# Clustered attention and two feed-forward layers on one core: moving the fourth product with V of each unit to the next step of TensorE

## What is computed

```python
# q, k, v: (2, 8, 768, 64); centroids: (8, 16, 64)
q_assign = argmax(einsum('bhsd,hcd->bhsc', q_n, c_n))      # nearest cluster of each query
k_assign = argmax(einsum('bhsd,hcd->bhsc', k_n, c_n))      # and of each key
mask = q_assign[:, :, :, None] == k_assign[:, :, None, :]
scores = where(mask, q @ k.T / sqrt(64), -1e9)
scores = scores - max(scores, axis=-1)
attn = exp(scores); attn = attn / (sum(attn, axis=-1) + 1e-9)
x = attn @ v                                               # then the two layers:
h = x @ w_in; g = P(h) / Q(h); y = g @ w_out               # moe,  d_ff = 2048
out = ((y @ w1) * (y @ w2)) @ w3 @ w_out                   # moe2, d_ff = 1024
```

## Time and profile before

| | us |
|---|---|
| median of 3 runs | 744.41 (744.14 to 745.87) |
| profiled execution, its time on the device | 743.99 |
| its span, first to last instruction | 742.2 |
| TensorE matmul busy | 721.5 (97%) |
| VectorE busy | 498.6 (67%) |
| ScalarE busy | 422.3 (57%) |
| GpSimd busy | 343.7 (46%) |
| TensorE's mean granted clock, share of full speed | 0.995 |

### The profile page before, as it was taken

The page is one execution under the profiler, slowest core; times in us unless marked ns, Lnnn a source line. Parts: engine busy times, 40 slices in busy tenths (PEclk is TensorE's granted clock), DMA queues, the critical chain, the costliest instruction groups (busy, mean ns, idle before and its releaser), DMA issues.

```text
span 742.2 us, 12733 instructions
## 1 busy us (share of the span) xinstructions
PE 721.5 (97%) x4849; PEld 591.2 (80%) x4849; DVE 498.6 (67%) x814; ACT 422.3 (57%) x750; POOL 343.7 (46%) x258
## 2 busy tenths in 40 slices
PE   4799999999999999999999999999999999999998
PEld 2467777777767788888888888878789999998886
DVE  6888888888855577677776777775876465543211
ACT  4366767666646888877767677764343322323221
POOL 5068787787875647642222224440204666451000
PEclk9899999999999999999999999999999999999999
DMA  7335645545421352000000032003101101000111
GB/s 159 72 89 129 157 112 150 145 114 151 104 55 39 115 162 68 0 1 1 0 1 1 0 114 103 11 29 89 54 30 29 30 29 56 2 1 23 49 43 57
DMA packets 66876, 47.75 MB, mean 64 GB/s; under 512 B 30528, under 2 KB 59136, under 8 KB 66816
## 3 DMA queue, kind: packets, MB, share of 16 engines
q1 hardware_dynamic: 66816, 46.95, 22.9%
HBM read 28.35 MB, written 3.15 MB: 42 GB/s over the span
## 4 chain that ended last, share of the span: by engine, by line
PE 91%; DVE 3%; SPq 2%; ACT 2%; DMA 1%; issue 1%; POOL 0%; DVEq 0%; ACTq 0%
PE psum L1156 89%; PE psum L1161 1%; DVE psum L1673 1%; DVE MROW L1673 1%; PE psum L688 1%; SPq L1095 1%; DVE OPS L1608 1%; DMA BQS<-NMT 1%; DMA RAWQK<-in_k 0%; ACT P L1452 0%; SPq L1078 0%; SPq L1055 0%; ACT OPS L1416 0%; DVE YS L884 0%; PE psum L1234 0%
## 5 line engine op out<-in xcount | busy, mean ns | idle before, releaser
L556 POOL TENSOR_TENSOR G<-TT,G 128x512 fp32r<-128x512 f32 x47 | 61.1, 1301 | 150.0 <-ACT G L435 150.0
L1838 POOL TENSOR_TENSOR PSUMS<-PSUMS,P 128x768 f32<-128x768 f32 x64 | 108.3, 1692 | 17.0 <-ACT P L1452 9.0
L1452 ACT ACTIVATE P<-psum 128x768 f32<-128x768 f32 x96 | 76.3, 809 | 46.5 <-PE psum L1156 46.1
L1673 DVE TENSOR_REDUCE psum<-psum 128x1 f32<-128x768 f32 x90 | 86.4, 960 | 19.7 <-PE psum L1156 18.8
L1156 PE MATMUL psum<-G,WSPLIT 128*128 128x512 f32 x360 | 86.8, 390 | 0.3 <-POOL G L556 0.3
L1156 PE MATMUL psum<-XT,WSPLIT 128*128 128x512 f32 x360 | 86.5, 389 | 0.0
L483 DVE SCALAR_TENSOR_TENSOR HH<-UU,ABSB,psum 128x512 f32<-128x512 f32 x48 | 35.9, 748 | 69.0 <-ACT TT L413 69.0
L1156 PEld LDWEIGHTS psum<-G,WSPLIT 128*128 128x128 f32 x360 | 67.3, 188 | 15.2 <-POOL G L556 0.9
L1156 PEld LDWEIGHTS psum<-XT,WSPLIT 128*128 128x128 f32 x360 | 67.6, 188 | 14.0
L1156 PE MATMUL psum<-P,V 128*32 128x194 f32 x1536 | 76.0, 332 | 0.1
L1156 PE MATMUL psum<-XT,SW 128*128 128x384 f32 x384 | 71.7, 334 | 0.0
(11 more groups left out here) (134 smaller groups left out, 1408.1 us busy)
## 6 DMA issues: line engine op xcount, KB each, us to landing
W3R<-in_moe_w SPq DMA_DIRECT2D x8, 512.0 KB, 3.7
RAWF<-in_moe_w SPq DMA_DIRECT2D x16, 256.0 KB, 3.3
RAWQK<-in_q SPq DMA_DIRECT2D x16, 192.0 KB, 3.2
RAWQK<-in_k SPq DMA_DIRECT2D x16, 192.0 KB, 3.9
BQS<-OPS SPq DMA_DIRECT2D x16, 192.0 KB, 2.8
OPS<-OPS SPq DMA_DIRECT2D x16, 192.0 KB, 3.0
V<-in_v SPq DMA_DIRECT2D x16, 192.0 KB, 2.6
XT<-XH SPq DMA_DIRECT2D x64, 48.0 KB, 2.0
```

Of the source, the lines that this page charges most:

```text
L556: nc.gpsimd.tensor_tensor(G[:, n % 2, 1, :], TT[:, n % 4, :], G[:, n % 2, 0, :].bitcast(F32), ALU.subtract).then_inc(g_lo, 1)
L1452: nc.scalar.activation(P32[:, (2 * u + n) % 4, :, 0:QS].rearrange("p (x y) n -> p x y n", x=2), score_banks(u, n).rearrange("p x (y n) -> ...
L1673: nc.vector.tensor_reduce(rows[:, n:n + 1], maxima_banks(u, n), AX.XY, ALU.max).then_inc(sm_free, 1)
L1838: nc.gpsimd.tensor_tensor(total, P32[:, (2 * u) % 4, :, 0:QS] if n == 1 else total, P32[:, (2 * u + n) % 4, :, 0:QS], ALU.add).then_inc(p_ ...
```

## The change

In TensorE's list, `probs_v(u, 3)` leaves the end of step u. It is issued in step u+1 instead, behind `scores(u + 1, 0)` and `score_max(u + 2, 3)` and directly in front of `probs_v(u, 4)`. For the last step its place is behind `scores(14, 0)`. No other engine's list is edited, and no wait, operand or size.

```diff
@@ -1338,6 +1338,8 @@
             def step(u):
                 scores(u, 0)
                 score_max(u + 1, 3)
+                if u > 1:
+                    probs_v(u - 1, 3)
                 probs_v(u - 1, 4)
                 probs_v(u - 1, 5)
                 sums(u - 1)
@@ -1359,12 +1361,12 @@
                 if has(u + 4):
                     sides(u + 4)
                 score_max(u + 2, 2)
-                probs_v(u, 3)
 
             for u in range(1, UNITS - 2):
                 step(u)
 
             scores(14, 0)
+            probs_v(13, 3)
             probs_v(13, 4)
             probs_v(13, 5)
             score_max(15, 3)
```

## The result

| | before | after |
|---|---|---|
| median of 6 runs, us | 744.47 (743.83 to 745.87) | 748.92 (747.94 to 751.73) |
| profiled execution, us | 743.99 | 749.49 |
| its span, us | 742.2 | 747.7 |

The ratio is 1.0059, with a 95% interval of 1.0049 to 1.0070: the change makes the kernel 4.45 us slower. Lines of the code behind the edit have moved by one or two: the reduction of `row_max` is L1675 now, the transpose of `turn_one_hot` L1670.

What follows compares the result with a forecast made beforehand. TensorE, busy 97% of the span, was taken to bound the kernel. Eleven boundaries at 0.30, plus 0.67, less 0.30 gave +3.67 us; 747.66 from the profiled run, forecast as 748.1 us, range 745.2 to 750.0.

Steps and rivals of the forecast that it cites:

- The new stretch: TensorE from score_max(u+2, 2) to sums(u): forecast 4.21 us against 3.91, so 0.30 us slower in each step.
- The chain by step 1: Step 1 already has this adjacency: 1.68 us between its two score_max, against 1.66 forecast for the new order.
- Part 1: TensorE's stretch to sums(u): grouping like products saves switches of shape, 3.61 us for 3.91, gaining 0.30 us a step.
- Part 2: At score_max(u+2, 3): the reduction loses its cover, so TensorE waits 0.50 us and restarts 0.10 us slower.
- The late landing: At scores(u+1, 0): one boundary in twelve has a late maxima DMA, taken to recur and cost 0.67 us.
- The last boundary: Step 13 to scores(14, 0): switches saved with no reduction in the way, -0.30 us.
- the eleven others: The boundaries without a late maxima DMA, each forecast to lose 0.30 us.
- The first: Rival at row_max(u+2, 2): the reduction doesn't bind, only switches count; 3.9 us won, 740.5 us; chance 0.08.
- the second: Rival at the same wait: it exists but is smaller; +1.0 to +2.2 us, 745.4 to 746.6; chance 0.17.
- The third: Rival at scores(u+1, 0): the maxima's DMA becomes the bound at every boundary; +7.7 us, 752.1; chance 0.06.
- the fourth: Rival on TensorE's clock: stalls lower it to 8 tenths, about 42 us, near 790; chance 0.01.

Runs made afterwards that it cites:

- experiment 1: Kernel after, with row_max(u, 2) of units 3 to 15 reducing only 192 of 768 columns: 743.72 us against 744.81, ratio 0.9986.
- experiment 2: Kernel before, with row_max(u, 2) shortened to 192 of 768 columns: 745.27 us against 744.81, ratio 1.0002.
- experiment 7: Kernel after with row_max(u, 2) shortened, and TensorE's wait for the maxima's DMA moved from scores(u+1, 0) to score_max(u+2, 2): 743.37 us against 744.78, ratio 0.9980.
- experiment 6: Kernel after, reordered: score_max(u+1, 3) behind the three products with V, scores and rest_of_k moved to match: 749.53 us, ratio 1.0058.
- experiment 9: Kernel after, whole, with only TensorE's wait for the maxima's DMA moved from scores(u+1, 0) to score_max(u+2, 2): 749.72 us against 745.15, ratio 1.0060.
- experiment 4: Kernel after, with VectorE's turn_one_hot(u+3) behind row_max(u+2, 2) instead of in front of it: 748.45 us, ratio 1.0048.

## Why the prediction was right, and where it was off

The direction, the mechanism and the size held: forecast 748.1 us (+3.67), measured 748.92 (+4.45 in the medians), and +3.5 in the trace from `sums(0)` on. The wait for `row_max(u + 2, 2)` is the cause: shortening that reduction alone takes the whole loss away (experiment 1), and does nothing where it is covered (experiment 2). Step by step:

- **The new stretch, 4.21 us against 3.91.** Measured 4.22. The chain by step 1 gave it: 1.68 us between the two `score_max` (1.66 to 1.68 forecast), then 0.55 (0.54), then 1.99 (2.01).
- **Part 1, fewer switches save 0.30 us.** This term failed. Experiment 1 shows 3.91 - 3.82 = 0.09. I took the pace of `score_max` into scores from another place of the step, 0.46; yet the earlier trace rows had the right pair: 43.55 to 44.18 are 0.63, behind a stall. And I took 0.70 for the scores, though the same working gave them 0.81 in this very place. Had nothing waited, the kernel would have been about 1.1 us faster, not 3.9.
- **Part 2, a wait of 0.50 and a restart of 0.10.** As the other term was too large, so was this one: between the two `score_max` it is 1.68 against 1.37 unhindered (113.04 - 111.67), a wait of 0.31, and the restart is 0.55 against 0.45. The two errors (0.21 and 0.19) cancel, since a stall ends when the reduction ends, however fast TensorE got there. The sum was safe; the split wasn't.
- **The late landing, +0.67 for one boundary.** It didn't recur. The trace after has no wait at `scores(u + 1, 0)`, so the twelve steps give 12 x (13.75 - 13.43) = 3.84 us, less the 0.27 by which the late landing had made one step before longer (13.70 for 13.43).
- **The last boundary, -0.30.** It gave 0.08. Before, it had been 3.70 us:

```profile
217.65 0.62 PE L1156 MATMUL psum<-OPS,BQS 128*128 128x384 f32 x2 [0.36 <-DVE psum L1673]
...
221.35 0.62 PE L1156 MATMUL psum<-OPS,BQS 128*128 128x384 f32 x2
```

and after it is 3.62:

```profile
223.24 0.62 PE L1156 MATMUL psum<-OPS,BQS 128*128 128x384 f32 x2 [0.36 <-DVE psum L1675]
223.88 0.59 PE L1156 MATMUL psum<-BQS,OPS 128*128 128x384 f32 x2
...
224.75 2.18 PE L1156 MATMUL psum<-P,V 128*32 128x194 f32 x48
226.86 0.62 PE L1156 MATMUL psum<-OPS,BQS 128*128 128x384 f32 x2
```

  So 3.84 - 0.27 - 0.08 = 3.49, the 3.5 in the trace. It is the same term of the switches, mis-sized. That my 3.67 is so near is in part luck: the late boundary lost 0.05, not 0.67, but the last gave 0.22 less than I had, and the eleven others lost 0.02 more each.
- **The rivals.** The first (no binding reduction, -3.9) is refuted by experiment 1 and by the trace; the second (a smaller loss, +1.0 to +2.2) by +3.5 in the trace and +4.45 in the medians. Its condition did half come true: the wait was smaller, but so was the saving against it. The third (the DMA at each boundary) is refuted by the list of waits; the fourth by the clock, which reads 1.00 in each window of 20 us from 40 to 260 in the kernel after, with a stall in each step. By the rule of the Trainium skill that I had named (TensorE: Matmul & The Clock Gate, "A second HAM failure mode: psum-queue depth-cycling") brief idling could have let it swing; stalls of 0.3 us in 13.75 didn't.
- **What stays open.** The medians differ by 4.45 us, the traces from `sums(0)` on by 3.5. The spread of the start (`sums(0)` at 47.1 to 49.2 us over the profiled executions of kernels in which nothing has moved up to there) is wide enough for the rest. The times go with the mean granted clock, if loosely: in the 20 executions of the kernel before beside experiment 1, the four at 0.986 took 745.8 to 747.0 us and the five at 0.995 took 743.6 to 744.6. After, the two at 0.986 took 749.49 and 751.73, the other four 747.9 to 749.3. For the six of before that stand in the table no clock is on record, so that the start makes the difference of the medians isn't shown.

## What to carry to other kernels

Before an instruction is moved, ask what it covers where it stands: here its own 0.8 us lay over a reduction whose bank the next product reuses, and TensorE's 97% busy share said nothing of it. Where a dependence closes the gap, the new time is the length of the dependence, so find one place in the trace in which it already binds and take the interval from there, rather than from a sum of paces. A saving by grouping like instructions is worth only what is left once every producer is again as far from its consumer as the slower engine needs.

## What the runs showed of the hardware

Going from one group to the next on TensorE has no one price. The same pair, `score_max` into scores, took 0.46 us from start to start in one place and 0.58 in another, without a stall in either; the weight load in the slower one starts 0.28 us late, and moving one of the two semaphore waits from in front of it gave back 0.11 (experiment 7). Two switches more, around a lone pair of matmuls between groups of 32 columns, cost 0.30 us (experiment 6).

A DMA can be far later in one execution than in others. In the profiled run of experiment 9 `score_max(8, 0)` stood for 3.5 us, once:

```profile
125.87 0.80 PE L1156 MATMUL psum<-OPS,BQS 128*128 128x384 f32 x2 [3.54 <-issue]
...
128.10 2.17 PE L1156 MATMUL psum<-P,V 128*32 128x194 f32 x32
```

The profile names no releaser, but `score_max(8, 0)` waits for the copies of unit 8's masks. The four that stand in SyncE's queue from 116 to 119 us landed after 2.5 to 7.6 us; the 48 of the kernel before from 60 to 240 us took at most 3.3:

```profile
DMA to landing us min/median/max: 2.5/2.9/7.6
```

```profile
DMA to landing us min/median/max: 1.9/2.5/3.3
```

The slowest was the last of the four. It was issued at about 118.15, so it landed near 125.8, where TensorE starts again. A load of 256 KB of weights that stands in front of it in the queue took 9.2 us, for 3.9 in the kernel before; what slowed both isn't shown. In experiment 4 the last of the same four copies took 5.2 us, and TensorE stood for 1.1.

Such a stall costs more than its length. TensorE was busy for 0.33 us of 122 to 124 and for 0.13 of 124 to 126, at a granted clock of 1.00 still. Then the clock read 0.52 from 126 to 128 and 0.63 from 128 to 130, so it was at its lower level (0.50, 1.2 GHz) for most of that time, and 1.00 again from 130. The work from this `score_max(8, 0)` to `score_max(8, 1)` took 4.33 us (125.87 to 130.20), for 2.81 one step earlier (108.50 to 111.31). With the stall that step was 5.1 us longer than its neighbours. The execution took 754.1 us, where the other five took 748.7 to 750.4. The 0.3 us stalls of the kernel after did nothing of the kind.
